# Shorter way of the last token tile to the first expert slot, fewer filler products, a third weight ring, and earlier register reads on ScalarE

## The reference

```
scores = q @ k.T / sqrt(64), window: 0 <= i - j < 64; x = softmax(scores) @ v     # tokens x 512
p = domain_probs / sum;  x = sum over 4 experts of p[:, e] * (relu(x @ w1[e]) @ w2[e])   # 512 -> 1024 -> 512
do = x @ w_skip > 0;  e_idx = argmax(x @ w_gate);  g = softmax(x @ w_gate)[e_idx]         # 8 experts
out = x + where(do, g * (relu(x @ u1[e_idx]) @ u2[e_idx]), 0)
```

## Time and profile before

| what | value |
|---|---|
| time, median of 3 runs | 636.95 us (636.81 to 636.97) |
| the profiled execution | 636.43 us, its span 634.8 us |
| TensorE busy | 622.9 us, 98% of the span |
| VectorE, ScalarE, GpSimd busy | 292.0, 245.3, 76.9 us |
| TensorE's granted clock | 0.998 of full speed over the span |
| transfers | 90.27 MB, 142 GB/s in the mean |

### The profile page before, as it was taken

The page is one execution under the profiler, slowest core; times in us unless marked ns, Lnnn a source line. Parts: engine busy times, 40 slices in busy tenths (PEclk is TensorE's granted clock), DMA queues, the critical chain, the costliest instruction groups (busy, mean ns, idle before and its releaser), DMA issues.

```text
span 634.8 us, 9772 instructions
## 1 busy us (share of the span) xinstructions
PE 622.9 (98%) x3469; PEld 554.4 (87%) x3470; DVE 292.0 (46%) x767; ACT 245.3 (39%) x518; POOL 76.9 (12%) x121
## 2 busy tenths in 40 slices
PE   8999999999999999999999999999999999999995
PEld 8888999898989898989899998989877788888884
DVE  5576556524512124512124334344467744771681
ACT  5775445422401013301113221322335754873771
POOL 6570000000000000000000001000011222231221
PEclk9999999999999999999999999999999999999999
DMA  8644133006999995310002331033347968693541
GB/s 277 187 130 149 38 112 133 36 1 213 215 261 227 247 248 202 87 45 0 0 0 66 100 102 74 1 129 99 117 135 241 373 196 267 192 363 82 162 159 22
DMA packets 51315, 90.27 MB, mean 142 GB/s; under 512 B 13129, under 2 KB 17737, under 8 KB 51281
## 3 DMA queue, kind: packets, MB, share of 16 engines
q1 hardware_dynamic: 47088, 82.15, 43.7%
q0 software_dynamic: 3520, 7.53, 4.6%
q10 hardware_dynamic: 672, 0.15, 0.1%
HBM read 64.15 MB, written 27.08 MB: 144 GB/s over the span
## 4 chain that ended last, share of the span: by engine, by line
PE 94%; DVE 3%; issue 1%; DMA 1%; ACT 1%; POOL 0%; ACTq 0%; SPq 0%; POOLq 0%; DVEq 0%
PE ps_h L1103 31%; PE ps_y L1103 29%; PE ps_y L1189 10%; PE ps_h L1189 10%; PE ps_s L1015 3%; PE ps_o L1060 2%; PE ps_s L1204 2%; PE ps_h L1003 2%; PE ps_t L1030 1%; PE ps_h L1127 1%; PE ps_s L1080 1%; DMA raw<-u 1%; PE ps_t L1178 1%; PE ps_t L1070 1%; ACT w_hi_a L581 0%
## 5 line engine op out<-in xcount | busy, mean ns | idle before, releaser
L669 ACT ACTIVATE ht_hi<-ps_h 128x384 fp32r<-128x384 f32 (+1 forms) x104 | 48.6, 467 | 235.8 <-PE ps_h L1103 228.9
L1103 PE MATMUL ps_h<-xt_hi,w_hi_a 128*128 128x384 f32 (+1 forms) x400 | 130.9, 327 | 0.0
L1103 PE MATMUL ps_h<-xt_hi,w_lo_a 128*128 128x384 f32 (+1 forms) x400 | 129.4, 323 | 0.0
L1103 PE MATMUL ps_h<-xt_lo,w_hi_a 128*128 128x384 f32 (+1 forms) x400 | 129.3, 323 | 0.0
L1103 PE MATMUL ps_y<-w_hi_a,ht_hi 128*128 128x512 f32 x288 | 115.6, 401 | 0.0
L1103 PE MATMUL ps_y<-w_hi_a,ht_lo 128*128 128x512 f32 x288 | 112.7, 391 | 0.0
L1103 PE MATMUL ps_y<-w_lo_a,ht_hi 128*128 128x512 f32 x288 | 112.4, 390 | 0.0
L890 DVE SCALAR_TENSOR_TENSOR ht_lo<-ps_h,ht_hi 128x384 fp32r<-128x384 f32 (+1 forms) x104 | 54.7, 526 | 118.8 <-ACT ht_hi L669 118.6
L1103 PEld LDWEIGHTS ps_h<-xt_hi,w_hi_a 128*128 128x128 f32 x400 | 75.4, 188 | 0.5 <-DVE ht_lo L890 0.2
L1103 PEld LDWEIGHTS ps_h<-xt_lo,w_hi_a 128*128 128x128 f32 x400 | 75.4, 188 | 0.4
L1103 PEld LDWEIGHTS ps_h<-xt_hi,w_lo_a 128*128 128x128 f32 x400 | 75.3, 188 | 0.0
(11 more groups left out here) (163 smaller groups left out, 837.8 us busy)
## 6 DMA issues: line engine op xcount, KB each, us to landing
raw<-u SPq DMA_DIRECT2D x40, 512.0 KB, 4.6
x_sorted<-xg SPq DMA_DIRECT2D x4, 4112.0 KB, 45.4
raw<-w SPq DMA_DIRECT2D x32, 512.0 KB, 4.6
x<-u SPq DMA_DIRECT2D x24, 512.0 KB, 5.9
vt<-v SPq DMA_DIRECT2D x17, 256.0 KB, 2.9
xg<-x_sorted POOLq DMA_DIRECT2D x13, 257.0 KB, 4.6
kt<-k SPq DMA_DIRECT2D x8, 384.0 KB, 5.2
x_sorted<-xg SPq DMA_DIRECT2D x1, 2313.0 KB, 43.7
```

Source lines behind the costliest of these rows:

```text
L669: a.activation(ht_hi[:, pos, 0:P * tiles], ps_h[:, pos % 2, 0:P * tiles], ACT.Relu).then_inc(h_hi_done, 1)
L1103: ins = mm(dst, hi_lo[l], rhs_hi_lo[r], start=(first and n == 0), stop=(last and n == 2))
```

## The change

1. FILL_FIRST goes from 13 to 9 and FILL from 2 to 1. In the tail one block of 3 fillers goes and one block of 3 stays.
2. The last tile goes in two halves of 256 columns. VectorE finishes it in two instructions with a semaphore after the first; TensorE transposes the halves into two banks (`ps_t`, `ps_y`), ScalarE copies them apart, and the logits' first two products need the first half alone. The gathered rows of slot 0 stand in two banks (`ps_o` for columns 0 to 255, `ps_h` for 256 to 511), and ScalarE and VectorE split them half by half (`turn_first_slot`). One of the four products of `early_rows` is moved behind the transpositions, and `take` of tiles 6 and 7 goes behind the logits and the count.
3. `dest_f` isn't made any more: `match` compares `slot_row` - `row_base` with `place_row`. For tile 8 the match comes ahead of the gate's two instructions and of `dest`. The logits' maximum is taken ahead of their copy.
4. Expert 1's second layer (`u2`, 1) lands in a third ring, `raw_third`, in memory that the dense stage held, once the last dense block h is made. The second layer of expert 0 is issued between and is no longer stuck behind the last tile's store: its last piece now stands ahead of `store(8)`. What `raw` gets next is expert 2's first layer.
5. ScalarE reads the number of slots of expert 0 ahead of slot 0, not after it, and copies weight piece 3 of expert 0's second layer after the first slot's rows.

```diff
-    FILL_FIRST, FILL = 13, 2
+    FILL_FIRST, FILL = 9, 1
...
-    TAIL = [("early_rows",), ("route", "turn", NT - 1), ("take", LATE), ("route", "logits", NT - 1)]
-    TAIL += [("take", LATE + 1), ("route", "rank", NT - 1), ("count",), ("fill", 3), ("take", NT - 1), ("fill", 3)]
+    TAIL = [("early_rows", range(0, 3)), ("route", "turn", NT - 1), ("early_rows", range(3, 4)), ("route", "logits", NT - 1)]
+    TAIL += [("take", LATE), ("route", "rank", NT - 1), ("count",), ("take", LATE + 1), ("take", NT - 1), ("fill", 3)]
...
-            for i in range(KC):
-                weights(u2, 0, (w1_split, E1 + 1), pieces=(i,))
-                if i < CT:
-                    store(2 * CT + i)
-            weights(u2, 1, (w2_split, E1))
-            weights(u1, 2, (w2_split, E1 + 1))
+
+            sp.wait_ge(h_ready, E1 * CHUNKS * FC + MORE_BLOCKS)
+            weights(u2, 1, pieces=(0, 1), ring=raw_third, landed=third_landed)
+            weights(u2, 0, (w1_split, E1 + 1), pieces=(0,))
+            weights(u2, 1, pieces=(2, 3), ring=raw_third, landed=third_landed)
+            weights(u2, 0, (w1_split, E1 + 1), pieces=(1,))
+            store(2 * CT)
+            weights(u2, 0, (w1_split, E1 + 1), pieces=(2,))
+            store(2 * CT + 1)
+            weights(u2, 0, (w1_split, E1 + 1), pieces=(3,))
+            store(2 * CT + 2)
+            weights(u1, 2, (w2_split, E1))
...
+                if stage == "turn" and t == NT - 1:
+
+                    act.wait_ge(last_half_turned, 1)
+                    act.wait_ge(logits_ready, t)
+                    copy(xr[:, 0:2, :].rearrange("p c n -> p (c n)"), ps_t[:, 0:2 * P]).then_inc(last_half_copied, 1)
+                    act.wait_ge(turned, t + 1)
+                    copy(xr[:, 2:4, :].rearrange("p c n -> p (c n)"), ps_y[:, t % 2, 0:2 * P]).then_inc(turned_copied, 1)
...
+            def turn_first_slot():
+                act.wait_ge(first_xs_half, 1)
+                copy(xs_hi[:, 0:2, :].rearrange("p c n -> p (c n)"), first_rows_half(0)).then_inc(first_xs_half_hi, 1)
+                act.wait_ge(xs_ready, 1)
+                copy(xs_hi[:, 2:4, :].rearrange("p c n -> p (c n)"), first_rows_half(1)).then_inc(xs_hi_done, 1)
...
                 if points is EXTRA_FIRST:
 
-                    slot(0, extra)
                     act.wait_ge(slots_ready, 1)
...
-                if points is EXTRA:
-                    slot(s0, extra)
+                slot(s0 if points is EXTRA else 0, extra)
...
             weights_hi(E1, KC + 2, 0)
+            turn_first_slot()
             weights_hi(E1, KC + 3, 0)
-            turn_slot(0, ps_o)
             routed(0, 0, True, EXTRA_FIRST)
...
                                                 scalar=0.0, op0=ALU.mult, op1=ALU.add, accum_out=place_row[:]))
-                    count(d.tensor_tensor(dest_f[:, t:t + 1], place_row[:], row_base[:], ALU.add))
+                    if t == NT - 1:
+                        match(t)
+                        gate(t)
                     d.tensor_tensor(dest[:, t:t + 1], place_row[:], row_base[:], ALU.add).then_inc(dest_ready, 1)
...
-                d.tensor_scalar(in_slot[:, t - LATE, :], slot_row[:], dest_f[:, t:t + 1], None,
-                                ALU.is_equal).then_inc(matched, 1)
+
+                d.tensor_scalar(in_slot[:, t - LATE, :], slot_row[:], row_base[:], place_row[:],
+                                ALU.subtract, ALU.is_equal).then_inc(matched, 1)
...
+                for i in range(2):
+                    own = slice(2 * i, 2 * i + 2)
+                    ins = minus_hi(xs_lo[:, own, :].rearrange("p c n -> p (c n)"), first_rows_half(i),
+                                   xs_hi[:, own, :].rearrange("p c n -> p (c n)"))
+                ins.then_inc(xs_split, 1)
```

More of the change, by code:

```diff
@@ L168, in build_block @@
         slot_row = sb("slot_row", [P, P])
-        sb("unused_a", [P, 144])
+        over = sb("over", [1, E2, E2])
+        sb("unused_a", [P, 80])
         raw = sb("raw", [P, RING, F])
@@ L202, in build_block @@
         dest = sb("dest", [P, NT], U32)
-        dest_f = sb("dest_f", [P, NT])
-        over = sb("over", [1, E2, E2])
+        sb("unused_d", [P, NT])
         n_slots = sb("n_slots", [1, E2])
@@ L255, in build_block @@
         more_landed = [sem(f"more_landed_{i}") for i in range(RING)]
+        third_landed = [sem(f"third_landed_{i}") for i in range(RING)]
         w1_hi_done, w1_split = sem("w1_hi_done"), sem("w1_split")
@@ L592, in weights_hi @@
                         ring, landed, h = raw_more, more_landed, g_no - (E1 + 2)
+                    elif isinstance(g_no, int) and g_no == E1 + 1:
+                        ring, landed, h = raw_third, third_landed, 0
                     else:
@@ L828, in attention, with gate @@
                             minus_hi(dst, src, outputs(xt_hi, r, j)[0]).then_inc(xt_split, 1)
+            def gate(t):
+                dve.wait_ge(gate_summed, t + 1)
+                link(d.tensor_scalar(gate_den[:], gate_sum[:], EPS, None, ALU.add))
+                link(d.reciprocal(x[:, t, D + 1:D + 2], gate_den[:]))
             def route(stage, t):
@@ L832, in route @@
                     dve.wait_ge(logits_ready, t + 1)
-                    count(d.tensor_copy(logits[:], ps_s[:, 0, 0:E2 + 1]))
-                    link(d.max(out=top[:], in_=ps_s[:, 0, 0:E2]))
+                    count(d.max(out=top[:], in_=ps_s[:, 0, 0:E2]))
+                    link(d.tensor_copy(logits[:], ps_s[:, 0, 0:E2 + 1]))
                     d.tensor_scalar(neg_top[:], top[:, 0:1], -1.0, None, ALU.mult).then_inc(top_ready, 1)
@@ L971, in _ @@
                     route(*what[1:])
-            match(NT - 1)
             dve.wait_ge(rank_ready, NT + 1)
@@ L1064, in route @@
             def route(stage, t):
-                if stage == "turn":
+                if stage == "turn" and t == NT - 1:
+                    pe.wait_ge(last_x_half, 1)
+                    pe.wait_ge(turned_copied, t)
+                    for c in range(KC // 2):
+                        last = turn(ps_t[:, P * c:P * c + P], x[:, t, P * c:P * c + P], ident[:])
+                    last.then_inc(last_half_turned, 1)
+                    pe.wait_ge(y_added, NT * (E1 - 1) + t + 1)
+                    for c in range(KC // 2, KC):
+                        n0 = P * (c - KC // 2)
+                        last = turn(ps_y[:, t % 2, n0:n0 + P], x[:, t, P * c:P * c + P], ident[:])
+                    last.then_inc(turned, 1)
+                elif stage == "turn":
                     pe.wait_ge(y_added, NT * (E1 - 1) + t + 1)
@@ L1154, in dense, with early_rows @@
                             beside(at, Y0 + FC * i + f)
-            def early_rows():
+            def early_rows(cs):
                 pe.wait_ge(early_landed, 16)
-                for c in range(KC):
-                    last = mm(ps_o[:, P * c:P * c + P], xg[:, P * c:P * c + P], ident[:], start=(c == 0), stop=False)
-                last.then_inc(early_taken, 1)
+                for c in cs:
+                    last = mm(first_rows(c), xg[:, P * c:P * c + P], ident[:], start=(c % (KC // 2) == 0), stop=False)
+                if cs[-1] == KC - 1:
+                    last.then_inc(early_taken, 1)
             def take(t):
@@ L1167, in take @@
                 for c in range(KC):
-                    last = mm(ps_o[:, P * c:P * c + P], x[:, t, P * c:P * c + P], in_slot[:, t - LATE, :],
-                              start=False, stop=(t == NT - 1 and c == KC - 1))
+                    last = mm(first_rows(c), x[:, t, P * c:P * c + P], in_slot[:, t - LATE, :],
+                              start=False, stop=(t == NT - 1 and c % (KC // 2) == KC // 2 - 1))
+                    if t == NT - 1 and c == KC // 2 - 1:
+                        last.then_inc(first_xs_half, 1)
                 if t == NT - 1:
@@ L1191, in passes, with slot, up @@
                 return ins
-            def slot(s, e, par):
-                def up(half, kcs, lo_ready=None):
+            def slot(s, e, par, first=False):
+                def up(half, kcs, lo_ready=None, meanwhile=None):
                     cols = slice(512 * half, 512 * half + 512)
@@ L1258, in routed @@
                     slot(s, e, par)
-            slot(0, 0, 0)
+            slot(0, 0, 0, True)
             pe.wait_ge(slots_ready, 1)
```

62 lines of the change are left out of this document (43 added, 19 removed).

## The result

The change makes the kernel 0.5% faster: 633.37 us in the median of 6 runs (632.62 to 634.98) against 636.88 before (6 runs, 635.49 to 636.97), ratio 0.9949 with a 95% interval of 0.9939 to 0.996. The forecast was 633.6 with a range of 632.2 to 635.5. The profiled execution is the slowest of the six, 634.98, and it matters why: its clock fell ahead of slot 0.

The account below looks back on a forecast made before the run. TensorE's own work bounds both long stages, so only prologue, tail and slot 1 could gain: 1.85 + 1.20 + 0.25 = 3.3 us. Profiled 636.43 becomes 633.1; the median, 0.52 above, 633.6 (range 632.2 to 635.5).

Parts of the forecast that it names:

- Start of the prologue: Prologue's start: with nine fillers, queries landing about 5.4 and clock rising at 7.15, second scores end 1.05 us earlier.
- Two of my own signs of a wrong prediction: Prologue: fillers or scores at 0.44 us a product behind 8 us; prologue's end moved by under 1 us.
- Middle and last steps: Prologue after its start: one filler less a step gives 0.45 us in four full steps, 0.35 in the last three.
- Prologue, sum: Whole prologue, up to the first dense product: 1.85 us earlier.
- bound elsewhere: Rival, prologue: ScalarE (6.16 of 6.75 us busy) or a late fourth piece bounds it; 0.5 instead of 1.85, 635.0; chance 0.13.
- the fourth: Prologue's fourth weight piece: lands at 17.5, wanted by ScalarE about 18.0; if later, ScalarE's queue would stand behind it.
- Tail: From the last dense product's end to slot 0's first product: 1.2 us shorter, bounds 0.3 to 1.55.
- slower: Rival, prologue: fewer fillers let TensorE fall to 1.2 GHz, 1.35 us lost a step, about 640 at worst; chance 0.04.
- Slot 1: Slot 1: ScalarE reads slot numbers once less, so TensorE's wait for `hs` shrinks; 0.25 us, at most 0.45.
- at nothing: Third ring's loads, issued during the last dense products, and expert 2's earlier first layer: counted as no gain or loss.
- The row load: Rival, slot 0: GpSimd's row load, sharing traffic with expert 2's second layer, lands 1.8 us late; total 635.4; chance 0.06.
- The halves: Rival, tail: splitting the last tile doesn't pay, more hand-overs and busy ScalarE; tail gains 0.3, total 634.5; chance 0.10.

Follow-up runs that it names:

- experiment 3: Changed kernel with one filler more ahead of the last tile's rank products and one ahead of the count: 632.74 us, ratio 0.9939.
- experiment 6: Changed kernel with ScalarE's reads of the slot numbers put back behind slot 0: 633.6 us, ratio 0.996.
- experiment 8: Changed kernel with `take` of tile 6 moved behind the count, leaving TensorE idle for longer: 635.95 us, ratio 0.9992.
- experiment 9: Changed kernel with 11 and 1 prologue fillers, first two weight copies one step later, and two fillers in the tail's idle stretches: 632.75 us, ratio 0.994.
- experiment 10: Kernel of experiment 8 with five fillers ahead of the rank products and one ahead of the count: 633.88 us, ratio 0.9956.
- experiment 11: Kernel of experiment 9 with the first weight piece issued ahead of tile 1's keys and queries: 633.12 us, ratio 0.9943.
- experiment 1: Kernel before with 9 and 1 fillers in place of 13 and 2, nothing else: 635.54 us, ratio 0.9986.
- experiment 7: Changed kernel with two rings instead of three, expert 1's second layer landing in `raw` behind `store(8)`: 634.41 us, ratio 0.9975.
- experiment 12: Kernel before, unchanged, run again for the mean clock of each execution: 636.58 us, ratio 0.9998.
- experiment 2: Changed kernel with the fillers put back to 13 and 2: 633.55 us, ratio 0.9951.
- experiment 4: Changed kernel with 11 fillers at the start instead of 9, still one in each step: 632.98 us, ratio 0.9937.
- experiment 5: Changed kernel with 11 and 1 fillers and the prologue's first two weight copies one step later: 633.33 us, ratio 0.9957.

## Why the prediction was right, and where it wasn't

**Start of the prologue: 1.05 predicted, 0.17 measured in the changed kernel's profile, the step that failed.** I fixed two moments that aren't fixed. The queries land not at 5.4: where the scores waited for them they started at 5.79 to 6.37 (changed kernel, experiments 3, 6 and 8 to 11), and the profile of the changed kernel gives 4.5 us to landing where I took 3.9 from the earlier trace rows. Experiments 1 and 7 had them by 5.3, after 3.6 us. And the clock doesn't rise at 7.15: in the profiled executions records of the fast pace begin anywhere between about 4 us (experiment 10, in the midst of the fillers) and 10.6 (experiment 3). Two of my own signs of a wrong prediction came true in the changed kernel's profile: scores at the low pace behind 8 us, and an end of the prologue that moved by under 1 us.

The first transposition of the probabilities is a good place to divide the prologue: in every trace the clock has risen by then or rises at it. Points of time in us; 13 and 2 are the fillers; the rise of the clock is my estimate from the durations of the rows.

| kernel | clock rises near | first transposition | from there to the first dense product |
|---|---|---|---|
| before; experiment 12 (13 and 2) | 7.1; 7.0 | 10.22; 10.11 | 13.72; 13.72 |
| experiment 2 (13 and 2) | 5.5 | 9.37 | 13.76 |
| changed kernel; experiment 3 (9 and 1) | 9.7; 10.6 | 10.05; 10.18 | 13.04; 13.04 |
| experiments 6; 8; 10 (9 and 1) | 7.0; 6; 4 | 9.44; 9.33; 9.31 | 12.99; 12.99; 13.00 |
| experiments 1; 7 (9 and 1) | 6.3; 5.0 | 8.87; 8.34 | 14.15; 14.16 |
| experiment 4 (11 and 1) | 7.1 | 9.68 | 13.24 |
| experiments 5; 9; 11 (11 and 1, later copies) | 5.7; 4.4; 5.8 | 9.04; 9.22; 9.51 | 13.27; 13.28; 13.28 |

The start is worth 0.04 to 0.17 where the clock rose late and 0.8 to 0.9 in experiments 6, 8 and 10. In experiments 1 and 7, where the queries were there by 5.3 too, it is 1.35 and 1.88, but the wait for the weight piece behind it takes 0.4 of that back. And an early rise alone brings as much with all fillers in place (experiment 2: 0.85). The rule of the Trainium skill that I cited ("TensorE: Matmul & The Clock Gate", the callout on the warm-up budget) is time under load and not a count, and the callout adds that the moment varies from run to run. This case agrees that a count doesn't set it: with the same fillers (9 and 1) the rise came anywhere from about 4 (experiment 10) to 10.6 (experiment 3). What sets it no run here shows.

**Middle and last steps: 0.80 predicted, 0.7 measured**, by the last column, where ScalarE waited for its first weight piece by 0.2 at most and the copies stand as before (13.72 to about 13.0). Where it waited over 1 us (experiments 1 and 7: 1.27 and 1.36) these steps took 0.4 more than before, and with the later copies they gain 0.45.

**Prologue, sum.** 1.85 predicted; 0.72 to 1.63 measured over the kernels with fewer fillers, 0.85 in the profiled execution. The rival "bound elsewhere" was partly right, and its bounds are other ones than it named: not ScalarE's share of 6.16 in 6.75 us but the landing of the queries and of the *first* weight piece, where I had feared the fourth. In experiments 1, 2, 4, 7 and 10 ScalarE waited 0.20 to 1.36 us for that piece; in 1 and 7 the scores also waited 0.36 and 0.45 for keys. By medians the fillers are worth 0.9 us alone (experiment 1, 0.14% of 636.65), 0.6 between experiments 2 and 4, and only 0.2 between experiment 2 and the changed kernel.

**Tail: 1.2 predicted, 1.24 measured** (8.60 to 7.36) in the profiles of experiments 2, 3, 4, 6, 7, 9 and 11 (7.34 to 7.36), and by its own steps: the logits start 1.83 us behind `early_rows` (469.05 to 470.88; predicted 469.89 to 471.72, the same 1.83), the count 4.76 (predicted 4.73), slot 0 7.36 in experiment 2 (predicted 7.4). In the changed kernel's own profile the clock ate it. I had priced a fall to 1.2 GHz, as the rival "slower", but looked for it in the prologue alone, where no trace shows one. The section that I cited there (the Trainium skill, "TensorE: Matmul & The Clock Gate", "HAM oscillation") tells of an engine that waits 3 to 5 us for a transfer before each group of products. It would not have pointed at the tail, where the stretches are 0.24 and 0.28 us, the second of them in the earlier trace rows already. This trace shows the same fall after these much shorter stretches, at a price of 1.62 us. What is new in the changed kernel isn't the idle time (0.52 us in the tail, before 0.83) but, among other things, what follows: two takes at once, where three fillers and one take stood.

**How often it falls.** I count a mean clock of 0.995 or less as a fall. The traces bear this out, as far as they go: the three with 0.995 (changed kernel, experiments 5 and 8) have the fall in the tail, the eleven with more have none. It is a sign and no proof, since the mean also takes in the end of the span, behind the last products (clock from 625 us on: 0.85 before, 0.64 in experiment 2). The changed kernel has 1 run of 6, experiment 5 two of 5, experiment 7 three of 9, experiments 2, 4 and 6 none of 15; together 6 of 35 with the changed tail and its gaps open, against 3 of 80 with the tail of before. On the chip of experiments 5 to 8 and 12 alone it is 5 of 19 against 1 of 45. So the change probably made falls more frequent (equal rates would give so uneven a count in one or two cases of 100), as theory B of experiment 12 says; the reason that B gives, takes in place of fillers, wasn't tried by itself. Longer gap (experiment 8), on that same chip: eleven of 11, which shows that idle time in this place goes with the fall. Gaps filled (experiments 3, 9, 10, 11): none of 20, but all of them ran on the other chip, where with open gaps (experiments 2 and 4) none of 10 fell either. That one filler a gap helps the changed kernel is therefore not shown by the counts; the medians (632.74 and 632.75 against 633.37) lean that way, but the intervals of the ratios overlap.

**Slot 1 and the third ring: 0.25 predicted, 0.94 measured** against the profile of before, 0.70 to 1.01 over the kernels with early reads. The stretch itself varies by 0.46 among the three traces with the slots of before (156.31, 156.61, 156.77), so the smaller terms are rough. The reads: I counted 0.25 where taking them out frees 0.78 of ScalarE, and their upper bound, the 0.45 by which TensorE was late, is what they bring against before (the row at 495.91 stands 0.92 behind the product ahead of it, after 0.45: 0.47). Of the rest 0.14 lies behind slot 1, unplaced, and 0.33 in slot 0: from its first product to slot 1's are 12.76 us before and 12.43 after. There I had put nothing. Before, ScalarE waited 0.88 us for a piece of expert 1's second layer and copied it at 486.21, ahead of `hs_hi`; after, it takes all four without a wait. Experiment 7 has 12.47 with two rings, so it isn't the third ring that brings this. The order of issue (no last piece behind the tile's store) is the likely cause; the other edits around slot 0 weren't tried apart. For the ring "at nothing" fits the profile of experiment 7 (155.61 against 155.37) and not its median, 1.0 us longer: open.

**The row load** wasn't late: it is issued at 479.31, `own_ids` are there at 483.91, and TensorE turns the rows at 488.18 without a wait. **The halves**: the rival's tail of 0.3 is refuted by the steps above. How much of the 1.24 is theirs and how much comes from moving `take` behind the logits, no run separates.

**Sum.** -0.85 + 0.38 - 0.94 + 0.01 = -1.4 in the profiled execution. Without the 1.62 of its fall it would be -3.0, a span of 631.8; the other five runs have spans of 631.0 to 632.2, and 631.5 was predicted. The median was right to 0.2 us because a prologue that I overrated by about 0.9 stood against slots that I underrated by 0.7: two sizes were off in opposite directions, and that the sum came out is luck. The rest doesn't add up neatly either: experiment 2 gains 3.1 us in the median with all fillers in place, where I had 1.45 for tail and slots. Its profile has 1.24 from the tail, 0.91 from the slots and 0.81 from the early rise of the clock. Whether the change makes that rise earlier or it was chance, no run shows. What holds of the mechanism is the tail, step by step, and the 0.7 of the middle steps.

## What to carry to other kernels

List TensorE's idle stretches on the predicted timeline, and price what stands behind each at both clocks; a dummy product in such a gap costs nothing while the engine would wait anyway (tail 7.36 with and without, experiments 3 and 2). Fillers ahead of a first product hide landings: before taking them out, look up in the trace when each of the next three or four loads lands, not the one that is asked for last. Judge a change at the start of a program by a point behind the rise of the clock, or by many executions: here one early rise moved the end of the prologue by 0.81, as much as the fewer fillers did in the changed kernel's profile (0.85). Read the price of a register read that gates an engine's instruction stream from the idle time in front of the next instruction (0.78 us less of it here), not from the read instructions' own (0.25).

## What the runs showed of the hardware

- After idle stretches of 0.24 and 0.28 us TensorE fell to 1.2 GHz in two traces (changed kernel, experiment 5) and, by the mean clock, in 6 runs of 35; after 1.23 and 0.28 in 11 of 11. The products at the low pace last from 473.94 to 477.38 in the changed kernel, and from 473.11 to 476.52 in experiment 8; either costs 1.6 us.
- At the start of the program the granted clock reads 1.00 while products take 0.43 us each, twice what they take later (0.22); only the durations tell of it. The moment of the rise differs between executions by up to 6.5 us.
- A transfer of 128 KB issued near 1.5 us lands after 3.6 to 4.8 us from one execution to the next, and after 3.9 and 4.4 in two executions of the kernel before. A load that seems hidden in one trace may not be in the next.
